# A delta-rule kernel: the transposed inverse is kept block-diagonal, and an update's first product is made of whole products

## The reference

```python
def _attn_ref(q, k, v, beta):            # 4 batches, 8 heads, 768 steps, head size 48
    k_n = k / (np.linalg.norm(k, axis=-1, keepdims=True) + 1e-06)
    state = np.zeros((B, H, D, D))
    for t in range(S):
        y[:, :, t] = np.einsum('bhd,bhde->bhe', q[:, :, t], state)
        v_old = np.einsum('bhde,bhd->bhe', state, kt)
        state = state + bt * np.einsum('bhd,bhe->bhde', kt, vt - v_old)

def _moe_ref(x, ...):                    # 3072 tokens, 384 wide, each to its best of 8 experts
    out[mask] = gate * eom * (np.maximum(x[mask] @ w1[e], 0) @ w2[e])

def _moe2_ref(x, w1, w2, w3, w_out):
    h = np.maximum(np.maximum(x @ w1, x @ w2), x @ w3)
    return h @ w_out
```

## Time and profile before

| | us |
|---|---|
| median of 3 runs | 1069.67 |
| lowest, highest | 1061.57, 1069.88 |
| profiled execution | 1061.8 |
| its span | 1060.1 |
| TensorE busy in the span | 1008.5 |
| VectorE busy | 522.3 |
| ScalarE busy | 375.6 |
| GpSimd busy | 364.0 |

### The profile page before, as it was taken

How to read it: one execution, slowest core, us unless ns; L and a number is a source line. 1 busy time by engine, 2 the same in 40 slices (tenths; PEclk the granted TensorE clock), 3 DMA queues, 4 the chain that set the end, 5 groups by cost and what they waited for, 6 DMA issues and landing times. The chain is left out here.

```text
span 1060.1 us, 28043 instructions
## 1 busy us (share of the span) xinstructions
PE 1008.5 (95%) x11748; PEld 883.5 (83%) x11748; DVE 522.3 (49%) x1109; ACT 375.6 (35%) x735; POOL 364.0 (34%) x275
## 2 busy tenths in 40 slices
PE   3899999999999999789999999998999999999998
PEld 3788888888888888669999999997788888888987
DVE  5567667775677765354444443442433333323332
ACT  3556566565566666122222222221312121212110
POOL 4545376554535342133564552634301010100000
PEclk9899999998999999689999999999999999999999
DMA  9222222221222120234542445322201010100000
GB/s 302 100 57 60 58 75 66 67 67 50 65 68 67 51 60 17 95 130 172 179 171 92 149 154 171 134 90 82 60 30 34 26 37 22 37 30 8 23 8 30
DMA packets 58044, 84.66 MB, mean 80 GB/s; under 512 B 28880, under 2 KB 52944, under 8 KB 55376
## 3 DMA queue, kind: packets, MB, share of 16 engines
q1 hardware_dynamic: 52272, 46.89, 14.3%
q0 software_dynamic: 5664, 36.18, 9.9%
HBM read 61.62 MB, written 21.43 MB: 78 GB/s over the span
## 5 line engine op out<-in xcount | busy, mean ns | idle before, releaser
L1159 PE MATMUL hb<-early,last_h 128*128 128x512 f32 x648 | 206.0, 399 | 0.5 <-DVE early L1303 0.5
L1159 PEld LDWEIGHTS hb<-early,last_h 128*128 128x128 f32 x648 | 120.4, 189 | 28.3 <-DVE early L1303 0.9
L1159 PE MATMUL hb<-early,last_l 128*128 128x512 f32 x324 | 128.4, 396 | 0.0
L750 POOL TENSOR_TENSOR n_base<-n_kb_a,cf 128x512 f16<-128x512 f32 x24 | 30.4, 1268 | 167.8 <-DVE n_kb_a L600 167.8
L610 DVE TENSOR_TENSOR p<-bank,cf 128x512 f16<-128x512 f32 x96 | 66.2, 690 | 36.0 <-PE bank L379 34.9
L552 ACT CAST t<-bank 128x512 f16<-128x512 f32 x96 | 56.5, 588 | 66.4 <-PE bank L372 66.1
L1196 POOL DMA_INDIRECT rows<-y_sorted,idx x24 | 24.5, 1022 | 155.1 <-PE ob L1227 151.8
L1159 PE MATMUL ob<-wo_h,early 128*128 128x384 f32 x288 | 75.1, 339 | 0.0
L1083 POOL TENSOR_TENSOR late<-w_raw,late 128x3072 fp32r<-128x3072 f32 x8 | 54.5, 6811 | 59.8 <-DVE late L1023 59.5
L1159 PEld LDWEIGHTS hb<-early,last_l 128*128 128x128 f32 x324 | 61.0, 188 | 14.8
L992 ACT CAST ht_h<-ht_bank 128x512 fp32r<-128x512 f32 x56 | 32.9, 587 | 109.4 <-PE ht_bank L943 55.4
(11 more groups left out here) (173 smaller groups left out, 2205.4 us busy)
## 6 DMA issues: line engine op xcount, KB each, us to landing
w_raw<-w POOLq DMA_DIRECT2D x14, 1536.0 KB, 7.7
kq_t<-qh SPq DMA_DIRECT2D x24, 256.0 KB
y_sorted<-y_sb SPq DMA_DIRECT2D x31, 192.0 KB, 1.9
x_in<-x_sorted SPq DMA_DIRECT2D x29, 192.0 KB, 2.5
k_raw<-kt_in SPq DMA_DIRECT2D x24, 192.0 KB, 2.4
v_in<-vh SPq DMA_DIRECT2D x24, 192.0 KB
k_own<-kh SPq DMA_DIRECT2D x24, 192.0 KB, 2.4
out<-o_sb SPq DMA_DIRECT2D x24, 192.0 KB, 1.8
```

The lines of the kernel that those rows point to most:

```text
L1159: ins = pe.matmul(out, a[x], b[y], start=first and i == 0, stop=last and i == 2, skip_group_check=True)
```

## The change

`tt16`, the fp16 copy of the transposed inverse, becomes block-diagonal: it has a further axis of two, and each half of the partitions writes only its own half of the columns; the rest is zero from a memset at the start. ScalarE copies partitions 0 to 63 and VectorE partitions 64 to 127, so `tt_out` counts two for each copy. The first product of an update becomes `both_heads`, eight whole products with that operand. The second product and the last product of `inv` stay as they are and read the diagonal blocks. `to_diagonal` on ScalarE only gathers the two copies that `both` already made.

```diff
-    tt16 = single("tt16", [P, U, C], F16)
+    tt16 = single("tt16", [P, U, 2, C], F16)
...
+            def tt(s, u):
+                return tt16[st][s, u, s.start // C, :]
...
             elif what == "update":
                 pe.wait_ge(prod_out[st], LVS * k + lv - LV0 + 1)
-                pe.wait_ge(tt_out[st], (LVS + 1) * k + lv - LV0 + 1)
+                pe.wait_ge(tt_out[st], 2 * ((LVS + 1) * k + lv - LV0 + 1))
                 pe.sem_inc(passed_pe, 1)
-                each_head(tt, pr, tb).then_inc(upd_done[st], 1)
+                both_heads(tt16[st], lambda u: p16[st][:, u, :], tb).then_inc(upd_done[st], 1)
                 each_head(pr, tt, ttb).then_inc(upd_done[st], 1)
...
             elif what == "inv":
-                pe.wait_ge(tt_out[st], (LVS + 1) * (k + 1))
+                pe.wait_ge(tt_out[st], 2 * (LVS + 1) * (k + 1))
...
     @block.scalar
...
             elif what == "turn":
                 act.wait_ge(turned_done[st], k + 1)
-                act.copy(tt16[st][:], ttb).then_inc(tt_out[st], 1)
+                act.copy(tt16[st][half[0], :, 0, :], ttb[half[0]]).then_inc(tt_out[st], 1)
             elif what == "update":
...
                 act.wait_ge(upd_done[st], 2 * (LVS * k + lv - LV0) + 2)
-                act.copy(tt16[st][:], ttb).then_inc(tt_out[st], 1)
+                act.copy(tt16[st][half[0], :, 0, :], ttb[half[0]]).then_inc(tt_out[st], 1)
...
     @block.vector
...
+            elif what == "turn":
+                dve.wait_ge(turned_done[st], k + 1)
+                dve.tensor_copy(tt16[st][half[1], :, 1, :], ttb[half[1]]).then_inc(tt_out[st], 1)
+            elif what == "update":
+                dve.wait_ge(upd_done[st], 2 * (LVS * k + lv - LV0) + 2)
+                dve.tensor_copy(tt16[st][half[1], :, 1, :], ttb[half[1]]).then_inc(tt_out[st], 1)
...
+            dve.memset(tt16[st][:], 0.0)
             dve.memset(z[st][:], 0.0)
```

More of the change, by code:

```diff
@@ L400, in inv @@
             tb, ttb, pb = bank[st]
-            nl, nb, t, tt, pr = (lambda s, u, x=x[st]: x[s, u, :] for x in (n_lo, n_base, t16, tt16, p16))
+            nl, nb, t, pr = (lambda s, u, x=x[st]: x[s, u, :] for x in (n_lo, n_base, t16, p16))
+            def tt(s, u):
+                return tt16[st][s, u, s.start // C, :]
             if what == "kt":
@@ L532, in _, with to_diagonal @@
     def _(act):
+        def to_diagonal(to, x):
+            for hh, s in enumerate(half):
+                ins = act.copy(to[s, :, hh, :], x[s])
+            return ins
         def inv(k, par, st, what, lv):
@@ L540, in inv @@
                 act.wait_ge(gram_out[st], 2 * k + 2)
-                for hh, s in enumerate(half):
-                    ins = act.copy(n_both[st][s, :, hh, :], n_kb_a[par][st][s, :, 0, :])
-                ins.then_inc(n_both_ready[st], 1)
+                to_diagonal(n_both[st], n_kb_a[par][st][:, :, 0, :]).then_inc(n_both_ready[st], 1)
             elif what == "high":
```

## The result

The changed kernel takes 1117.58 us (median of 4 runs, 1114.97 to 1121.6) against 1068.18 for the kernel before (4 runs beside it, 1061.57 to 1069.88): a ratio of 1.0506, 95% interval 1.0448 to 1.0564. The forecast was slower, 1093 within 1073 to 1114. The direction came true; the loss, about 50 us, is twice the 27 us worked out. In the profiled executions the span went from 1060.1 to 1117.1 us.

A forecast was written before the change was run, and what follows sets the result against it. TensorE's instruction stream was taken to set the pace. Form +6, issue -1, late copies +22 and memsets +1, less about 1, gave +27 us: 1089 on the profile, 1097 on the median; forecast 1093, range 1073 to 1114.

The forecast's parts named there:

- (a): Slot 6: two VectorE copies stand ahead of the product for update 2, which starts 0.65 us later a step.
- (b): Behind slot 6: stream 0's update 2 copy stands ahead of L607, delaying the last inverse product by 0.26 us a step.
- (c): Slot 9: update 3's copy waits ahead of the norm, `rhs` and L610, so update 4 starts 1.15 us later.
- (d): Copies of updates 4 and 5, in looser places of VectorE's order: 0.1 us a step allowed.
- list of signs: What profiles should show: TensorE waits naming VectorE's `p`, about 0.65, 0.26 and 1.15 us, once a step each.
- The first product: Each update on TensorE: eight whole products for sixteen small ones; changes of form cost 0.5 us a step, +6 us.
- Copies: ScalarE's halved copies gain or lose nothing; VectorE's 120 new ones take 0.69 us each.
- Memsets: Two new memsets at the start, before VectorE's first reduction: +1 us.
- The rival of the clock: Attention part: waits halve TensorE's clock in half of the steps, +16 us, 1105 on the profile's scale; chance 0.18.
- the hidden case: VectorE's new copies fit its 10.4 us idle a step and hide: 1068 on the profile's scale; chance 0.14.
- A second term: TensorE's stalls on "issue" shorten with 128 fewer instructions a step: -1 us, between 0 and -4.
- The rival of the instruction supply: TensorE's "issue" stalls go, up to -8.8 us, whole groups get cheaper, copies hide: 1055; chance 0.05.

The follow-up runs named there:

- e1: Changed kernel with each update's first product again sixteen 64 by 64 products, copies still shared by VectorE and ScalarE: 1094.44 us, +3.5% against the kernel before.
- e8: Kernel before, with two 512-column products into a free bank ahead of each wait of the last step: 1059.19 us, ratio 1.0008.
- e7: Changed kernel as it is, run again for a second profile: 1099.23 us, +3.76% against the kernel before.
- e9: Changed kernel as it is, run beside its two parts on another chip: 1117.28 us, +5.4% against the kernel before.
- e2: Changed kernel with ScalarE making both halves of the copies and VectorE none, whole first products kept: 1082.77 us, +1.9% against the kernel before.
- e11: Repeat of e2 in a later session on another chip: 1074.62 us, +1.3% against the kernel before.
- e10: Repeat of e1 in a later session on another chip: 1096.93 us, +3.3% against the kernel before.
- e3: Changed kernel with all of VectorE's copies of the updates put at the end of their slot: 1107.83 us.
- e4: Changed kernel with zero-operand products on TensorE, three ahead of stream 0's update 2 and five ahead of its update 4: 1098.06 us.
- e6: Changed kernel with eight more zero-operand products behind the first product of stream 0's update 4: 1094.25 us.

## Why the prediction was right in direction and too small

- *VectorE's copies are late*: right. (a) +0.65 forecast, +0.75 to 0.8 measured; (b) +0.26, +0.21 to 0.27; (c) +1.15, +1.26 (3.06 us from the Gram products in e1 too, with no change of form there, so none is hidden in it); (d) 0.1, nothing at stream 0's update 5. The excess of (a) and (c) is in the main one number: a mask product or norm operation starts 0.72 us after the copy ahead of it (284.63 to 285.35, 291.56 to 292.28), where I took 0.61. e1 charges the waits alone at 23 us over the kernel, against 22 forecast. That they name VectorE's `p` was in the list of signs and is there.
- *The first product*: 0.32 us forecast with the change of form as 0.33, measured 0.32 to 0.34. Without VectorE's copies the form costs 0.2 to 0.3 us a step against the kernel before and 0.6 against the same half steps in e8, 2 to 6 us where 6 stood.
- *Copies*: 120 casts, 695 and 692 ns (0.69 forecast); ScalarE's half, 580 ns against 598 for the whole bank: nothing gained, as said. *Memsets*: +0.62 us against +1. *After attention nothing moves*: 602 and 603 us.
- *The failed step*: the sum stopped at waits and change of form and left the clock at its old level, a term of nothing. The half clock from 45 us to the last Gram group grew by 37.5 us (10.2 to 47.8), in which about half of the work is lost (a stretch of 6.7 us lost 3), so 17 to 19 us; the half steps took 18.6 us more than the waits explain. Another 5.5 us went in the tail, where the half clock grew by 12. That is the missing half in this profile. It is not a fixed part of the loss: e7, the same kernel, had 27.3 us of half clock, a tail of 53.7 us and half steps with 3 us beyond the waits, e9 51.2, 51.1 and 20.
- *The rival of the clock*, with a chance of 0.18 ("if half of the steps lose the clock, +16 us: 1105 on the profile's scale"), was right in its place, behind (c), for half of it: seven stretches of 3.4 us where it had five or six of 6.7, some 12 us for its 16. The rest came behind stalls on "issue", which it left out. What I held against it was that thirteen waits of L372, up to 1.2 us, stand in the stretch and most did not bring the clock down. That count misled: ten of the thirteen are 0.3 us long, at one fixed place. Of the three waits of 0.9 us or more in that stretch (0.94, 1.23 and 1.29 us, on any line) two brought the clock down. And the change makes the update's products whole at the very place where the new wait arises: behind (c) the clock fell in 15 of about 30 steps with whole products and in 1 of 20 with small ones. I had priced the two parts one by one; that they act on each other shows in this count and not in the times.
- *The range* stopped at the clock case, 1114, and the measured 1117.58 lies past it; its lower end, 1073, was meant to lie just above the hidden case on the median's scale, but 1068 on the profile's scale is 1076 there.
- *A second term, not confirmed*: fewer instructions, "-1 us, between 0 and -4". Without waits "issue" is 11.6 to 12.8 us with the whole products against 8.8 before; with the waits it is 6.5 to 11.3 against 16.8 and 17.1 with small ones. So the runs give both signs, and the change as a whole gained nothing here (9.7). The stalls became fewer and longer: before, ten of 0.3 us stood at one fixed place, and two were over 1.2 us; with the form alone six are, in each of e2 and e11, and nine of these twelve had a stretch of half clock begin within 3.6 us of their start. The rival of the instruction supply (1055) fell with it.
- *Hidden copies* (0.14) fell: TensorE waits 18.5 us for VectorE.

**What stays open.** What the stalls on "issue" are. They cut a group in the middle (e2 above), and stand at nearly the same places in two profiles of one kernel (1.19 us ahead of 147.3 in e2 and of 144.3 in e11, 1.30 ahead of 202.8 and of 201.3; 2.47 and 2.28 us in both e1 and e10), so they belong to places in the instruction stream; every edit here moved that stream, and no run holds them still while it changes the form. Their sum goes neither with the number of instructions (e1 has as many as the kernel before and 16.8 us) nor with the form (e3 17.9, e4 9.4). Whether whole and parts differ at all is not decided either (the whole is 0.8% more on one chip, 1.7% less on the other), nor why the changed kernel came at 1.038 once and at 1.051 and 1.054 otherwise, while the small products came at 1.035 and 1.033; its profiles differ in the half clock, 27.3 against 47.8 and 51.2 us.

## What to carry to other kernels

Before giving a busy-time-idle engine more work, follow its own queue for one period: 6.1 us of copies fitted in 10.4 us of idle time, and still held TensorE up for about 2 us a step, because two of them stood ahead of a product without slack and one waited at the head of the queue with work behind it; moved to ScalarE at four places, the same copies cost no wait. And where a new wait lands on TensorE, give its clock a term in the sum, from the rows: list the waits by length before counting how many left the clock alone. Here the same 1.1 us wait cost 3, 5 or 7 of ten steps their clock with eight whole products behind it, and 0 or 1 of ten with sixteen small ones.

## What was not expected of the hardware

- Eight whole 64-column products and sixteen 64 by 64 ones take the same time from start to start (0.25 us, apart from the change of form), yet behind a wait of 1.1 us the granted clock fell to 0.50 in 15 of some 30 steps with the first and in one of 20 with the second.
- Eight more such products (0.23 us) behind the same wait kept the clock at full in all ten steps; the kernel e6, with more work in it than the changed one, was no slower than that on its chip (1094.25 against 1099.23).
- Stalls of 1.2 to 2.7 us inside a group of matmuls, released by nothing that the profile shows, at places that repeat in two profiles of the same kernel.
- A stretch of half clock of 3.4 us behind (c) cost more than its own half: in the changed kernel's first profile each of the seven was followed, some eight us after (c), by one more wait of about 0.8 us for VectorE (L617), and such a half step took 18.1 us for 16.1. In e9 it was so in three of three, in e7 that wait was 0.17 us and the half step 17.5.
